# GpSimd's key copies with a spread factor, and the means of V turned one step later on TensorE

## The reference

```python
k_sum = k.reshape(B, H, nb, block, D).max(axis=3)
v_sum = v.reshape(B, H, nb, block, D).mean(axis=3)
scores_l = scale * np.matmul(q, k.transpose(0, 1, 3, 2))
mask_l = np.abs(pos[:, None] - pos[None, :]) < window
scores_s = scale * np.einsum('bhsd,bhnd->bhsn', q, k_sum)
scores_s = scores_s + np.log(block)
scores_all = np.concatenate([np.where(mask_l, scores_l, -1e9), scores_s], axis=-1)
a = softmax(scores_all)
out = np.matmul(a, np.concatenate([v, v_sum], axis=2))
```

## Time and profile before

| what | value |
|---|---|
| median of 3 runs | 436.69 us |
| profiled execution | 435.59 us |
| its span | 433.8 us |
| PE busy | 424.6 us (98%) |
| DVE busy | 288.8 us (67%) |
| ACT busy | 226.9 us (52%) |
| POOL busy | 144.6 us (33%) |
| L652, the 18 key copies on POOL | 21.1 us, mean 1184 ns |
| PE's share of the chain that ended last | 88% |

### The profile page before, as it was taken

The page is one execution under the profiler, slowest core; times in us unless marked ns, Lnnn a source line. Parts: engine busy times, 40 slices in busy tenths (PEclk is TensorE's granted clock), DMA queues, the critical chain, the costliest instruction groups (busy, mean ns, idle before and its releaser), DMA issues.

```text
span 433.8 us, 8342 instructions
## 1 busy us (share of the span) xinstructions
PE 424.6 (98%) x3222; PEld 362.5 (84%) x3222; DVE 288.8 (67%) x518; ACT 226.9 (52%) x581; POOL 144.6 (33%) x162
## 2 busy tenths in 40 slices
PE   8889999999999999999999999999999999999997
PEld 3669996887777899778877988898998899889885
DVE  5974469875497546876867875767665875565353
ACT  7994577773279746777846452444443323324120
POOL 5999826100247320002293574323112022200000
PEclk9999999999999999999999999999999999999999
DMA  8974460000880400000231013113213252301103
GB/s 293 362 239 116 152 239 2 2 2 0 293 310 16 158 2 1 2 0 2 69 113 64 2 48 98 48 50 97 58 40 97 95 176 71 97 0 50 48 2 145
DMA packets 14799, 39.66 MB, mean 91 GB/s; under 512 B 1656, under 2 KB 3368, under 8 KB 14760
## 3 DMA queue, kind: packets, MB, share of 16 engines
q1 hardware_dynamic: 14328, 38.60, 26.6%
q10 hardware_dynamic: 432, 0.52, 0.3%
HBM read 33.56 MB, written 4.72 MB: 88 GB/s over the span
## 4 chain that ended last, share of the span: by engine, by line
PE 88%; DMA 3%; ACT 3%; POOL 2%; SPq 1%; issue 1%; DVE 0%; DVEq 0%
PE ps_s L780 35%; PE ps_o L780 19%; PE ps_x L780 15%; PE ps_t L780 11%; PE ps_t L958 4%; ACT PA L1209 2%; DMA VW<-in_vw 2%; DMA raw<-in_wv 1%; PE ps_t L852 1%; POOL PA L617 1%; PE ps_x L975 1%; POOL wv_l L636 1%; ACT PTA L1243 0%; PE ps_s L1049 0%; PE ps_x L1049 0%
## 5 line engine op out<-in xcount | busy, mean ns | idle before, releaser
L1461 ACT ACTIVATE HID_h<-HID_raw 128x384 fp32r<-128x384 f32 x48 | 25.1, 525 | 72.3 <-DVE HID_raw L1819 31.9
L723 POOL TENSOR_TENSOR W_raw<-W_raw 128x256 f32<-128x256 f32 x11 | 11.5, 1049 | 98.1 <-DMA W_raw<-in_ch 88.1
L780 PE MATMUL ps_s<-C_h,HID_l 128*128 128x512 f32 x96 | 37.8, 393 | 0.0
L780 PE MATMUL ps_s<-C_l,HID_h 128*128 128x512 f32 x96 | 37.7, 393 | 0.0
L780 PE MATMUL ps_s<-C_h,HID_h 128*128 128x512 f32 x96 | 37.6, 392 | 0.0
L1209 ACT ACTIVATE PA<-ps_s,nmaxA 128x120 f32<-128x120 f32 x96 | 34.1, 406 | 6.3 <-DVE nmaxA L1482 6.1
L1575 DVE TENSOR_REDUCE nmaxM<-ps_s 128x1 f32<-128x640 f32 (+5 forms) x28 | 26.7, 955 | 12.4 <-PE ps_s L780 12.3
L1808 DVE SCALAR_TENSOR_TENSOR HID_l<-HID_raw,HID_h 128x384 fp32r<-128x384 f32 x48 | 28.0, 588 | 10.4 <-ACT HID_h L1461 8.1
L780 PE MATMUL ps_o<-V_h,W_h 128*128 128x384 f32 x96 | 32.8, 342 | 0.1
L1281 ACT ACTIVATE PM<-ps_s,nmaxM 128x128 f32<-128x128 f32 (+5 forms) x48 | 30.1, 634 | 5.3 <-DVE nmaxM L1575 5.0
L780 PE MATMUL ps_o<-V_h,W_l 128*128 128x384 f32 x96 | 32.4, 337 | 0.0
(11 more groups left out here) (255 smaller groups left out, 1243.1 us busy)
## 6 DMA issues: line engine op xcount, KB each, us to landing
VW<-in_vw SPq DMA_DIRECT2D x12, 512.0 KB, 7.3
W_raw<-in_ch SPq DMA_DIRECT2D x12, 512.0 KB, 3.6
C_raw<-in_ch SPq DMA_DIRECT2D x12, 512.0 KB, 3.9
VT<-in_vT SPq DMA_DIRECT2D x8, 384.0 KB, 7.2
out_x<-US SPq DMA_DIRECT2D x11, 256.0 KB, 2.3
QT<-in_qT SPq DMA_DIRECT2D x7, 384.0 KB, 6.8
KP<-in_kT SPq DMA_DIRECT2D x6, 384.0 KB, 7.0
raw<-in_tok SPq DMA_DIRECT2D x4, 384.0 KB, 3.2
```

What stands on the lines that cost most here:

```text
L723: pool.tensor_tensor(W[S3], W[A11], W[A21], ALU.subtract).then_inc(w_sum, 1)
L780: return pe.matmul(out, lhsT, rhs, start=start, stop=stop)
L1461: act.activation(*own(s, n, half), ACT.Relu).then_inc(g_hi, 1)
```

## The change

Two edits that have nothing to do with each other.

**Key copies.** A column `factor` of 128x1 is filled once with `SCALE` by DVE at the start. POOL's 18 key copies are `tensor_tensor` multiplications with this column spread over 4 x 96, and no longer `tensor_scalar` with a number. POOL waits once for the column (`c_factor`) ahead of its first key copy.

**Means on TensorE.** In batch 0 the first means are turned in step k = 4, behind the scores of unit 4, and no longer in step k = 3 ahead of them. In both batches the second means are turned in step k = 8 behind the values of unit 4, and no longer ahead of them. ACT's list is as it was.

```diff
+        factor = sb("factor", [P, 1], F32)
...
-                pool.tensor_scalar(KW[:, r, 4 * i:4 * i + 4, 0:WK], windows(r, 4 * i), SCALE, None,
-                                   ALU.mult).then_inc(a_kwin, 1)
+                pool.tensor_tensor(KW[:, r, 4 * i:4 * i + 4, 0:WK], windows(r, 4 * i),
+                                   factor[:, :].unsqueeze(2).broadcast_to([P, 4, WK]), ALU.mult).then_inc(a_kwin, 1)
...
+            pool.wait_ge(c_factor, 1)
             key_copies(0, -1)
...
                     if k < NU:
                         a_scores(b, k)
+                    if b == 0 and k == 4:
+                        a_first_means(b)
 
                     if k <= NU + 2:
                         a_transpose(b, k - 3)
-                    if k == MEANS_AT:
-                        a_second_means(b)
-                    if b == 0 and k == 3:
-                        a_first_means(b)
                     if k == NU:
                         m_value(b, 0)
                     if k >= 4:
                         a_values(b, k - 4)
+                    if k == MEANS_AT:
+                        a_second_means(b)
...
+            dve.memset(factor[:, :], SCALE).then_inc(c_factor, 1)
```

More of the change, by code:

```diff
@@ L304, in program @@
         c_pool = sem("c_pool")
-        c_warm = sem("c_warm"); c_mask = sem("c_mask"); c_rows = sem("c_rows")
+        c_warm = sem("c_warm"); c_factor = sem("c_factor"); c_mask = sem("c_mask"); c_rows = sem("c_rows")
         ld_qt = sem("ld_qt")
```

## The result

| | before | after |
|---|---|---|
| median of 20 runs each | 436.68 us | 437.88 us |
| ratio of the times | | 1.003 [1.0018, 1.0042] |
| profiled execution, its span | 435.59, 433.8 | 437.86, 436.1 |
| POOL's 18 key copies | 21.1 us, mean 1184 ns | 14.6 us, mean 828 ns |

The account below looks back on a forecast made before the run. PE, 98% busy, was taken to bound the kernel, with ACT setting the pace in batch 1's attention. POOL's -0.33 and batch 1's means' +0.37 summed to +0.04 us, forecast 436.7 us, range 435.9 to 437.8.

Parts of the forecast that it names:

- The copies' price: POOL's key copies: a two-input copy takes 0.84 us, not 1.184, cheaper by 0.33 us each.
- Most of this is hidden: Of POOL's 18 cheaper copies, batch 1's twelve and five of batch 0's six change nothing at the end; one counts.
- rival 3: POOL's two-input copy is dearer, 1.68 us (+0.50 each), PE's transposes in batch 0 come 1.9 late: 439.0 us; chance 0.07.
- -0.33 at 30.96: Batch 0, unit 9's transposes on PE: POOL hands over at 30.63, so what follows shifts by -0.33 us.
- Part two: First means of batch 0, behind unit 4's scores: VS and ACT's queue 0.17 us later, a cost and no gain.
- Part three: Second means of batch 0, behind unit 4's values: VS 0.25 later plus 0.17, only 0.06 left behind a late load.
- Part four: Second means of batch 1, behind unit 4's values: VS 0.37 us later, ACT sets the pace, cost +0.37.
- Rival 1: PE's waits of 0.51, 0.59 and 0.42 us simply vanish, 1.5 gained in all: 435.2 us; chance 0.14.
- Rival 2: The means' delays are not absorbed, 0.17 + 0.25 in batch 0, 0.67 in batch 1, no POOL gain: +1.1, 437.8; chance 0.14.

Follow-up runs that it names:

- a2: The kernel before with only the 18 key copies made two-input, the factor in unused room of another tile, means as before: 436.9 us, ratio 1.0014.
- b2: The kernel before with only the six key copies between the attentions made two-input, the other twelve one-input, means as before: 437.26 us, ratio 1.0027.
- b1: The kernel before with twelve key copies made two-input, the six between the attentions left one-input, means as before: 436.17 us, ratio 0.9999.
- b4: b2 with POOL holding the six two-input copies until DVE has made the weights of unit 1: 436.5 us, ratio 1.0005.
- a1: The kernel before with an unused tile where the changed kernel has its factor column, no instruction added or moved: 436.76 us, ratio 0.9991.
- c2: The kernel before with only batch 1's second means moved behind the values of unit 4, copies as before: 437.1 us, ratio 1.0004.
- b3: The kernel before with a POOL memset that shifts the six one-input copies between the attentions against DVE: 436.81 us, ratio 1.0006.
- c3: The kernel before with all 18 copies two-input, the six between the attentions held as in b4, means as before: 436.42 us, ratio 0.9997.
- c4: The changed kernel with the six copies between the attentions held as in b4: 438.08 us, ratio 1.0024.
- a4: The changed kernel with its factor column in unused room of a small tile, so that no address moves: 438.7 us, ratio 1.0053.

## Why the prediction was wrong

The forecast was 436.7 us in a range of 435.9 to 437.8, with 0.84 on no measurable change; the result is 437.88.

- **The copies' price: right.** 0.828 us against 0.84 forecast. The 1.7 us that I set against it was no fault of the page. The Trainium skill ("GPSIMD Engine Reference", section "Performance versus the Vector engine") gives about 2.6 cycles an element for a `tensor_tensor`, and counts 1.2 GHz. Taken as they stand, these figures give an estimate of 384 x 2.6 / 1.2 = 832 ns, and the trace agrees. I had scaled the old copy's 1184 ns by 2.6 / 1.8, as if `tensor_scalar` ran at the page's best case; it took 3.1 ns an element.
- **"Most of this is hidden": the step that failed.** I let the twelve copies for batch 1 cost nothing because POOL had time, and gave as the reason the row of batch 1's attention. Six of the twelve don't stand there but at 65 to 72 us, in the second layer of batch 0, and I had read no row of that place. The question was not whether POOL had time but whom its instructions hold up: these six lie beside DVE's weights of the second layer and cost 0.80 to 0.85 us (a2, b2 and the changed kernel); taken back (b1) or moved (b4) the loss is gone. None of the four rivals had it: rival 3 made POOL late, and POOL was early. The trace of before showed the pattern in batch 1's second layer, beside POOL's two-input `column_sums`:

```profile
215.48 0.55 DVE L1590 TENSOR_SCALAR denM<-sumM 128x4 f32<-128x4 f32 x1
...
216.27 0.81 DVE L1601 TENSOR_TENSOR raw<-denM,gate_w 128x256 f32<-128x256 f32 x1
```

  I had not looked for the spread of one DVE line's durations.
- **-0.33 at 30.96: right only under a condition.** Take the time from the start of ACT's second `VW` in batch 0 to the first projection. With one-input copies it is 7.09 us in the kernel before and 7.08 in b2, with two-input copies 6.79 in a2, where the load of V was early: a gain of 0.3. But 6.79 is also what kernels with one-input copies show when that load is later (a1 6.79, c2 6.79, b3 6.80): POOL's gain is worth nothing then. The changed kernel's profile, with `VW` at 25.51, is such a case and shows 6.79 as well. In the 14 kernels' profiles `VW` idled 0 to 1.97 us for that load. I had taken one landing, 24.2, for fixed.
- **Part two: right.** Measured from the scores of unit 1, the first `VS` is 6.16 us behind in place of 6.03: +0.13 against 0.17 forecast, and the scores still waited 0.71 for ACT at unit 5.
- **Part three: right in kind.** The second `VS` came 0.16 later on that scale (16.75 us behind in place of 16.59, against 0.25 forecast), and the load covered it. PE's wait for `vsum` went over into one for ACT (1.25).
- **Part four: right in kind, too small.** +0.51 against +0.37. From the start of the transposes to that of the values it takes 0.59 us (138.16 to 138.75 in the changed kernel), to that of the means it took 0.49 (136.38 to 136.87 before); this 0.10 I had left out. `VS` came 0.49 later behind the transposes (1.72 us in place of 1.23).
- **The rivals.** Rival 1 fell: PE's three waits went and nothing was gained. Rival 2 gave the nearest number, 437.8, for another reason: delays of 0.5 and 0.8, one of them not among its own. Rival 3's price, 1.68 us, came from the mean of L706. That mean has a hold-up in it, as far as the timeline tells: in the kernel before three of its six instructions take 0.74 us, as L705 does, and the longest takes 2.53, from 269.55, while a two-input product of DVE (L1681) runs from 269.24 to 271.48; L706 ends 0.6 us after it. So the row that I took for a price was very likely a sign of what I missed, with the engines the other way round.

In sum: +0.8 for the six copies, +0.5 for batch 1's means, and 0 to -0.3 for the other copies, 1.0 to 1.3 us. The medians differ by 1.2, and the ratio says 1.3 [0.8, 1.8]. What the move of batch 0's means costs is not in this sum and stays open.

## What to carry to other kernels

A faster GpSimd instruction is not free because GpSimd has slack: list which VectorE instructions run beside it, and compare each one's longest duration in the trace with its shortest. A small instruction that sometimes takes three times as long, at the same shape, may be held up (`denM`, 0.16 to 0.55 us in the kernel before); moving GpSimd's instruction away tells. A mean that mixes both is no price. Keep GpSimd's instructions with two inputs away from VectorE's small steps on TensorE's path, or put a wait ahead of them, as in b4. Where a pacing engine is full, moving its producer back by one piece of work costs that piece, less what the pacing engine had still to do: here 0.76 us back, 0.27 still to do, 0.49 lost.

## What the runs showed of the hardware

A product of 128x384 with a column spread over it took GpSimd 0.83 us, the same copy times a number 1.18: the form with more inputs was the cheaper by 30%. A one-input GpSimd copy held up VectorE's `tensor_scalar` of 128x4 to its end (0.48 us instead of 0.18, in b3 alone) and left a two-input product nearly alone (0.48 instead of 0.43), while the two-input copy held up both (0.70 and 0.79). It is not the spread column that does it: plain two-input products of GpSimd held them up as much (0.55 and 0.81 at 215 us). VectorE's reciprocal of 128x4 (0.18), its copy from PSUM (0.68) and its reductions took the same time beside either. VectorE seems to hold up GpSimd too: one GpSimd product of 128x256 took 2.53 us beside a long one of VectorE, and 0.74 at its shortest; no run tested this. Of three executions in which TensorE waited 2.0 to 2.3 us for ACT near 28 us, the one that waited 2.03 (c3) kept its clock, and those of 2.16 (c4) and 2.26 (a4) show 0.92 for the stretch from 12 to 34 us; three executions make no rule.
